# The second attention's scores as one product of 128 partitions a head, and steps of one form side by side

## The reference, cut to what matters

```python
def _attn_ref(q, k, v, p):            # q, k, v: (4, 8, 576, 64); p: (4, 8, 32, 64)
    def sm_attn(qq, kk, vv):
        s = scale * np.matmul(qq, kk.transpose(0, 1, 3, 2))
        s = s - np.max(s, axis=-1, keepdims=True)
        a = np.exp(s)
        a = a / (np.sum(a, axis=-1, keepdims=True) + 1e-09)
        return np.matmul(a, vv)
    p_packed = sm_attn(p, k, v)           # first attention: 32 rows a head
    out = sm_attn(q, p_packed, p_packed)  # second: 576 rows a head against those 32
```

## Time and profile before

| what | value |
|---|---|
| runs, median (lowest to highest of 3) | 1705.7 us (1705.32 to 1707.46) |
| the profiled execution: its time; its span | 1704.49 us; 1702.7 us |
| busy share: PE, PEld, DVE, ACT, POOL | 99%, 88%, 74%, 43%, 74% |
| chain of work that ended last, by engine | PE 94%, POOL 2%, all others 1% or less |
| TensorE's granted clock, 40 slices | 9 in every slice (nine tenths of full or more) |
| waits of PE in the first 110 us | one of 1.1 us for the first data, three of 0.4 to 0.7 for ScalarE's results, one of 0.5 for nothing shown, one of 0.2 |
| DMA issues: k_raw, q_raw, v_raw | 512 KB each, 5.8 to 6.7 us to landing |

### The profile page before, as it was taken

How to read it: one execution, slowest core, us unless ns; L and a number is a source line. 1 busy time by engine, 2 the same in 40 slices (tenths; PEclk the granted TensorE clock), 3 DMA queues, 4 the chain that set the end, 5 groups by cost and what they waited for, 6 DMA issues and landing times.

```text
span 1702.7 us, 28100 instructions
## 1 busy us (share of the span) xinstructions
PE 1691.0 (99%) x10353; PEld 1491.6 (88%) x10353; DVE 1253.8 (74%) x2269; ACT 736.0 (43%) x1666; POOL 1253.5 (74%) x1384
## 2 busy tenths in 40 slices
PE   9999999999999999999999999999999999999999
PEld 7888888888888888888888888888888999889997
DVE  4846645787778787778787878787887677766776
ACT  5644466445444444445444545454532222232222
POOL 1256669987888888778888887888877985399650
PEclk9999999999999999999999999999999999999999
DMA  9431111111111211111112111111100011121101
GB/s 277 124 85 38 41 48 26 38 38 50 38 37 38 61 39 38 39 49 38 38 39 62 38 38 46 42 38 38 50 27 25 26 63 50 38 92 40 62 26 56
DMA packets 78390, 88.32 MB, mean 52 GB/s; under 512 B 8368, under 2 KB 63664, under 8 KB 78256
## 3 DMA queue, kind: packets, MB, share of 16 engines
q1 hardware_dynamic: 78256, 86.54, 18.9%
HBM read 81.81 MB, written 4.72 MB: 51 GB/s over the span
## 4 chain that ended last, share of the span: by engine, by line
PE 94%; POOL 2%; DMA 1%; ACT 1%; DVE 1%; SPq 1%; issue 0%; POOLq 0%; DVEq 0%
PE PS L1651 92%; PE PS L1671 2%; ACT g_raw L892 1%; DMA stage<-moe_w_dram 0%; POOL w_lo L643 0%; PE PS L1881 0%; DMA k_tail<-k_dram 0%; SPq L514 0%; DVE acc L1352 0%; POOL span_late L732 0%; POOL w_hi L641 0%; POOL recombined L716 0%; SPq L538 0%; POOL sums_of_a L724 0%; SPq L531 0%
## 5 line engine op out<-in xcount | busy, mean ns | idle before, releaser
L1651 PE MATMUL PS<-w_hi,h_hi 128*128 128x512 f32 x1440 | 565.7, 393 | 1.2 <-DVE h_lo L1583 0.6
L1651 PE MATMUL PS<-w_lo,h_hi 128*128 128x512 f32 x1440 | 563.4, 391 | 0.0
L1651 PE MATMUL PS<-w_hi,h_lo 128*128 128x512 f32 x1440 | 560.6, 389 | 0.0
L1357 DVE SCALAR_TENSOR_TENSOR acc<-PS,gate,acc 128x512 f32<-128x512 f32 x504 | 378.3, 751 | 178.9 <-PE PS L1651 178.9
L892 ACT ACTIVATE g_raw<-PS 32x256 f32<-32x256 f32 x992 | 373.3, 376 | 12.8 <-PE PS L1651 0.8
L1651 PEld LDWEIGHTS PS<-w_hi,h_lo 128*128 128x128 f32 x1440 | 270.4, 188 | 58.6
L1651 PEld LDWEIGHTS PS<-w_hi,h_hi 128*128 128x128 f32 x1440 | 270.8, 188 | 51.1 <-DVE h_lo L1583 1.1
L1651 PEld LDWEIGHTS PS<-w_lo,h_hi 128*128 128x128 f32 x1440 | 270.9, 188 | 45.8
L1108 ACT ACTIVATE h_hi<-PS 128x576 fp32r<-128x576 f32 x216 | 129.0, 649 | 303.4 <-DVE PS L1493 303.4
L1651 PE MATMUL PS<-a_parts,g_slots 128*128 128x288 f32 x1296 | 225.1, 295 | 0.2 <-POOL g_slots L764 0.2
L1651 PEld LDWEIGHTS PS<-a_parts,g_slots 128*128 128x128 f32 x1296 | 195.7, 188 | 9.6 <-POOL g_slots L764 0.6
(11 more groups left out here) (181 smaller groups left out, 2315.4 us busy)
## 6 DMA issues: line engine op xcount, KB each, us to landing
stage<-moe_w_dram SPq DMA_DIRECT2D x96, 512.0 KB, 4.8
stage<-moe_w_in_dram SPq DMA_DIRECT2D x32, 256.0 KB, 2.8
stage<-moe_w_out_dram SPq DMA_DIRECT2D x16, 512.0 KB, 3.6
k_raw<-k_dram SPq DMA_DIRECT2D x8, 512.0 KB, 6.3
q_raw<-q_dram SPq DMA_DIRECT2D x8, 512.0 KB, 5.8
v_raw<-v_dram SPq DMA_DIRECT2D x8, 512.0 KB, 6.7
out_dram<-acc SPq DMA_DIRECT2D x16, 256.0 KB, 3.7
p_twice<-p_dram SPq DMA_DIRECT2D x8, 64.0 KB, 4.7
```

The lines of the kernel that those rows point to most:

```text
L1357: return nc.vector.scalar_tensor_tensor(out=dst, in0=y, scalar=share, in1=dst, op0=ALU.mult, op1=ALU.add)
L1651: return nc.tensor.matmul(dst, lhsT, rhs, start=start, stop=stop)
```

## The change

- `ppT` grows from 256 to 512 columns, [head, r, 32]. It is zeroed once by GpSimd (`zeros_ready`), and then only rows 0 to 63 of r = 0 and rows 64 to 127 of r = 1 are written, by two copies of ScalarE in place of one. So one product of 128 rows with 64 columns gives both groups of tokens of a head, the zeros keeping them apart: `scores2` issues 8 products a chunk for c = 0, 1 where it issued 16. The tail keeps its form.
- Its results lie in one bank instead of across two, and the bank alternates between 4 and 5, so that a product waits for the scores of two chunks ago.
- `packed`: the second quad of heads begins with its tail product, right behind the first quad's.
- Six steps of TensorE's order are moved.

```diff
-        ppT = [sb(f"ppT{i}", [P, QUADS * P], scope=attn) for i in range(2)]
+        ppT = [sb(f"ppT{i}", [P, H, 2, NPACK], scope=attn) for i in range(2)]
...
-        TR, S1B, S2B, PPB = (0, 1, 6), 2, 4, 7
+        TR, S1B, S2B, PPB = (0, 1, 6), 2, (4, 5), 7
...
+            for i in range(2):
+                nc.gpsimd.memset(ppT[i][:], 0.0).then_inc(zeros_ready, 1)
...
             def packed_values(b):
-                evacuate("pp", b, 0, ppT[b % 2][:], lambda bank_: bank_[:, 0:QUADS * P])
+                unit = UNITS.index(("pp", b, 0))
+                for r in range(2):
+                    rows = slice(r * HALF, (r + 1) * HALF)
+                    done = copy(ppT[b % 2][rows, :, r, :],
+                                full(unit)[rows, 0:QUADS * P].rearrange("d (h n) -> d h n", n=NPACK))
+                done.then_inc(evacuated(unit), 1)
...
+            act.wait_ge(zeros_ready, 2)
             packed_values(0)
...
                 for Q in range(QUADS):
-                    for j in range(RUN + 1):
+                    order = [*range(RUN), RUN] if Q == 0 else [RUN, *range(RUN)]
+                    for j in order:
...
-                elif n:
+                elif b == B - 1:
                     pe.wait_ge(s2_taken, n)
-                copies = 4 if c < NC - 1 else 1
-                for step in range(H):
+                elif n >= 2:
+                    pe.wait_ge(s2_taken, n - 1)
+                for h in range(H):
+                    if c < NC - 1:
+                        last = mm(bank(s2_bank(b, c))[0:tokens, :].rearrange("s (r h n) -> s r h n", r=2, h=H)[:, :, h, :],
+                                  qT[i][:, h, col:col + tokens], ppT[i][:, h, :, :])
+                        continue
                     for r in range(2):
-                        h = step if r else H - 1 - step
                         rows = slice(r * HALF, (r + 1) * HALF)
...
```

The moves in TensorE's order:

```diff
             turn_k(1, 3)
+            turn_k(1, 4)
             packed_gates(0)
-            turn_k(1, 4)
             scores1(1, 0)
...
             turn_k(2, 0)
+            scores2(0, 1)
             turn_q(1, 4)
-            scores2(0, 1)
             turn_k(2, 5)
...
             turn_p(2)
+            turn_k(2, 4)
             turn_k(2, 2)
-            turn_k(2, 4)
             turn_q(2, 5)
             turn_packed(1)
...
             turn_k(3, 5)
+            turn_q(3, 5)
             scores2(2, 0)
-            turn_q(3, 5)
             turn_q(3, 0)
             turn_a(1, 1)
             scores1(3, 1)
+            packed_gates(2)
             turn_q(3, 1)
-            packed_gates(2)
             scores2(2, 1)
```

More of the change, by code:

```diff
@@ L216, in attention_moe_mlp @@
         consts_ready, ones_ready = sem("consts_ready"), sem("ones_ready")
+        zeros_ready = sem("zeros_ready")
         v_in = sem("v_in")
@@ L390, in attention_moe_mlp @@
         TURNED_UNITS = """
[L391 to L394, removed]
+            p00 k00 k02 k01 k05 k03 k04 q02 q03 e00 q00 e01 e02 q01 q04 q05 p10 k12 k11 pp00 k10
+            k13 k14 k15 q15 q12 q13 q10 k20 q14 k25 e10 q11 e11 e12 k23 k21 p20 k24 k22 q25 pp10
+            a00 q23 q24 q22 a01 q21 e20 e21 e22 q20 p30 a02 k32 k31 k30 k34 pp20 k33 a10 k35 q35
+            q30 a11 q31 e30 e31 q32 e32 q33 q34 a12 a20 pp30 a21 a22 a30 a31 a32
         """.split()
@@ L437, in s2_bank @@
         def s2_bank(b, c):
-            return LAST_S2B[c] if b == B - 1 else S2B
+            return LAST_S2B[c] if b == B - 1 else S2B[(b * NC + c) % 2]
         def scores2_of(b, c):
-            at = s2_bank(b, c) * BANK + BANK - H * NPACK
             _, rows, groups = PARTS[c]
+            at = s2_bank(b, c) * BANK + (BANK - H * NPACK if c == NC - 1 else 0)
             return PS[0:rows, at:at + groups * NPACK].rearrange("s (h n) -> s h n", n=NPACK)
@@ L941, in hi_of_packed @@
                 copy(pp_parts[0:HALF, :, b * NPACK:(b + 1) * NPACK],
-                     ppT[b % 2][0:HALF, :].rearrange("d (h n) -> d h n", n=NPACK)).then_inc(pp_hi_ready, 1)
+                     ppT[b % 2][0:HALF, :, 0, :]).then_inc(pp_hi_ready, 1)
             def p_part(b):
@@ L1285, in lo_of_packed @@
                 nc.vector.tensor_tensor(
-                    pp_parts[HALF:P, :, cols], ppT[b % 2][0:HALF, :].rearrange("d (h n) -> d h n", n=NPACK),
+                    pp_parts[HALF:P, :, cols], ppT[b % 2][0:HALF, :, 0, :],
                     pp_parts[0:HALF, :, cols].bitcast(F32), ALU.subtract).then_inc(pp_split, 1)
@@ L1739, in packed @@
                                 weights_, values = e1T[i][0:2 * TAIL, QUADS * RUN + Q, cols], tail[:, h, :]
-                            last = mm(bank(PPB)[out_rows, Q * D:(Q + 1) * D], weights_, values, j == 0, j == RUN)
+                            last = mm(bank(PPB)[out_rows, Q * D:(Q + 1) * D], weights_, values, j == order[0], j == order[-1])
                 last.then_inc(pp_full, 1)
@@ L1755, in scores2 @@
                     pe.wait_ge(s2_taken, n - 1)
-                elif n:
+                elif b == B - 1:
                     pe.wait_ge(s2_taken, n)
-                copies = 4 if c < NC - 1 else 1
-                for step in range(H):
+                elif n >= 2:
[5 more added lines that the diff above has]
+                        continue
                     for r in range(2):
-                        h = step if r else H - 1 - step
                         rows = slice(r * HALF, (r + 1) * HALF)
[L1765 to L1773, removed]
+                        at = (s2_bank(b, c) + 1) * BANK + (h - H) * NPACK
+                        last = mm(PS[r * TAIL:(r + 1) * TAIL, at:at + NPACK], qT[i][rows, h, col:col + tokens],
+                                  ppT[i][rows, h, r, :])
                 last.then_inc(s2_full, 1)
@@ L1833, in packed_gates @@
                         last = mm(bank(GWB)[hq * NPACK:(hq + 1) * NPACK, Q * E:(Q + 1) * E],
-                                  ppT[b % 2][rows, h * NPACK:(h + 1) * NPACK], wg_raw[rows, h // 2, :])
+                                  ppT[b % 2][rows, h, hq % 2, :], wg_raw[rows, h // 2, :])
                 last.then_inc(gw_full, 1)
```

## The result

| | median | runs | range |
|---|---|---|---|
| before | 1705.31 us | 22 | 1703.97 to 1708.38 |
| after | 1710.03 us | 22 | 1705.43 to 1714.96 |

The ratio is 1.0026, with a 95% interval of 1.0020 to 1.0032: slower by just over the 0.2% that can be told apart, and 3 us above the range. The profiled execution of after took 1711.15 us, with a span of 1709.4 against 1702.7.

What follows compares the result with a forecast made beforehand. TensorE, busy 99% of the span, was taken as the bound. Terms of 0.74 + 0.35 + 0.22 + 0.48 − 0.05 − 0.23 + 0.05 + 0.27 = 1.83 us saved gave 1703.9 us, range 1700.0 to 1707.0.

Steps and rivals of the forecast that it cites:

- The sum: All priced changes in the attention's TensorE steps added together: 1.83 us saved.
- a pass of the new form: In the second score product, a full-height pass takes 0.11 us, set by loading 128 weight columns.
- scores2(0, 0) and (1, 1) with their neighbours: Second score products between full-height transpositions: 1.87 us instead of 2.24, saving 0.37 us each, nearly all switches of form.
- wait of q35: Transposition turn_q(3, 5), now ahead of scores2(2, 0), waits 0.57 us for VectorE's copy of k33; net 0.23 us longer.
- k24 and pp10: turn_k(2, 4) before turn_k(2, 2): adjacent tails save 0.27 us of switches, but a wait for ScalarE's copy leaves 0.05.
- each half copy of `ppT`: ScalarE copies in two halves: 0.38 us becomes 0.38 + about 0.26, four times, hidden but for k14.
- if nothing else is late behind it: Condition on the bound: taking TensorE time away can pay in full, provided no other work arrives late.
- No DMA is added or moved: Check of data loads: none changes, and loads that follow TensorE's steps follow them earlier; no cost counted.
- The rival of the clock: Fewer columns moved in scores2 could drop TensorE to 1.2 GHz in the attention; 16 us of it gives 1712; chance 0.05.
- Moved columns as the pace: Rival: moved columns, not weight loads, pace the new product at 0.06 us a pass, giving 1697.5 us; chance 0.10.
- No wait is felt: Rival: q35, pp10 and the early steps cost nothing; 2.8 to 3.2 us saved, about 1702.8 us; chance 0.13.
- The change doesn't do what it says: Rival: switches at each edge, 0.12 us or more a pass, or felt ScalarE copies; about 1706 us; chance 0.12.

Runs made afterwards that it cites:

- the padded version: After with a warm-up of 8 large and 26 small products instead of 10 large, moving later TensorE instructions by 96 records: 1704.46 us, ratio 0.9991.

## Why the prediction was wrong

**The sum was right.** The profile of after moved by 96 records has no pause marked "issue" and no half clock in the attention. It checks the sum, in distances of starts:

| step | forecast | measured |
|---|---|---|
| a pass of the new form | 0.11 | 0.108 |
| scores2(0, 0) and (1, 1) with their neighbours, each less than before | 0.37 | 0.39 |
| scores2(0, 1) with its neighbours | 2.89 | 2.87 |
| scores2(2, 1), gates, scores1 | 3.03 | 2.98 |
| scores2(1, 0) | 2.18 | 2.19 |
| wait of q35 | 0.57 | 0.55 |
| scores2(3, 0) and (3, 1), more than before | 0.05 | 0.09 |
| packed(2), less than before | 0.09 | 0.13 |
| from turn_p(2) to scores1(2, 0) (k24 and pp10), less than before | 0.05 | −0.01 |

Two of the rows behind this, from its timeline, answer to the earlier trace rows: 30.78 − 27.91 = 2.87 us, the tails now side by side.

```profile
27.91 0.60 PE L1684 MATMUL PS<-ident,k_raw 128*128 128x128 f32 x4
28.35 1.90 PE L1661 MATMUL PS<-ppT,acc 128*128 128x64 f32 x16
30.18 0.43 PE L1684 MATMUL PS<-ident,q_tail 32*128 32x32 f32 x4
30.45 0.41 PE L1684 MATMUL PS<-ident,k_tail 32*128 32x32 f32 x4
30.78 0.66 PE L1684 MATMUL PS<-ident,second 128*128 128x128 f32 x4
```

The weight loads of scores2(0, 0) in after show the price of a pass and the missing switches: 27.31 − 25.58 = 1.73 us for 16, with no idle time on either side, where the earlier trace rows have 1.99 and a switch.

```profile
25.20 0.42 PEld L1681 LDWEIGHTS PS<-ident,q_raw 128*128 128x128 f32 x4
25.58 1.87 PEld L1661 LDWEIGHTS PS<-ppT,acc 128*128 128x128 f32 x16
27.31 0.48 PEld L1681 LDWEIGHTS PS<-ident,q_raw 128*128 128x128 f32 x4
```

The Trainium skill, TensorEngine Tiling (Array Packing), "When to Use Tiling", wants two row tiles for a contraction of 64. The prediction worked out from it that here the two forms come out even. The trace agrees but for the switches: 0.108 us a pass here, 0.112 us a pair before.

From the tail k15 to the first product of the experts the padded version takes 50.89 us (23.40 to 74.29), before 53.08 (22.14, to 75.22): 2.19 less. Of these, 0.54 is a pause that before has and this one lacks (66.31 to 67.21, against 65.71 to 66.07), and 1.65 is the change. The sum said 1.83.

One term was mis-sized without harm: each half copy of `ppT` takes 0.378 us (8 of them in after), as long as the whole copy did, so the second adds 0.38 us and not 0.26. It stayed hidden.

**The step that failed** is the sentence "if nothing else is late behind it", which the prediction then checked for banks, copies and data loads only: "No DMA is added or moved". The queue that brings instructions was never looked at, though the page lists it, and before's own timeline has one of its pauses at 66.5 us, which the table ahead of the prediction gives as a wait "for nothing shown". It was taken as a price already paid:

```profile
66.31 0.43 PE L1671 MATMUL PS<-ident,q_tail 32*128 32x32 f32 x4
67.21 0.31 PE L1671 MATMUL PS<-ident,second 64*128 64x64 f32 x2 [0.46 <-issue]
```

It is number 2241 = 193 + 8 × 256. An edit that leaves out 128 passes and their loads moves the later borders, by up to one block; at `packed(1)`, with two chunks of second scores behind it, by 64 records. What stands in place of "nothing else is late" is a stop of 1.73 us in `packed(1)` (2.0 us in the account) and 10.2 us at half clock behind it (4.0 us).

**The rival of the clock** (chance 0.05) named the right mechanism of the loss and the wrong trigger. It put the fall down to fewer columns moved; the runs show it behind a pause. Its price was near: 10.2 us at half clock, halved, are 5.1, and the account shows 4.0 between the starts of scores1(2, 0) and scores1(2, 1), without the first 1.1 us of the stretch. It was to decide from 10.5 us on; the pause's own 2 us made it decide with less. "Against: the clock stays at 1.00 through waits of up to 0.7 us" was true and no evidence for a pause of 1.7 us.

**Moved columns as the pace** (chance 0.10) is refuted by 0.108 us a pass. **No wait is felt** is refuted: q35 waits 0.55 us. **The change doesn't do what it says** is refuted by the table.

**The chances.** 0.08 for slower was too little. What stays open: what sets how long after a border the next packet begins. It was at once before (number 705 at 28.38, the packet at 28.35) and 3.8 to 5.9 us later ahead of the six such pauses of 1.59 us and more. Data loads alone don't explain it. In before the DMA engines were full when that packet began at once, and carried nothing at all while the packet behind number 2241 (66.52) took until 69.32:

```profile
28.00:28.40 0.40, 0.40 (x9) 0.40 (x10) 0.40 (x2) 0.40 (x2) 0.00 (x0) 1.00 1.27 358
66.55:69.30 2.75, 2.29 (x32) 1.59 (x34) 2.30 (x9) 1.43 (x4) 2.00 (x3) 1.00 0.00 0
```

So the place of a harmful border can be found in a trace, but not forecast from the code with what is shown here.

## What to carry to other kernels

Where a stream of short instructions (here 256 in 4.4 us) keeps TensorE full, look in the profile for idle time put down to "issue" in the middle of a loop, and compare it with the packets of the instruction queue; an edit that changes the number of instructions then has to be timed at two or three shifts of the stream (dead instructions at the start), or the shift is measured and not the edit. The versions of after span 7.4 us over shifts alone (those of before 6.1), over four times the change's own worth; before itself had medians of 1704.6 to 1706.3 us in the same sets of runs. The best of after (1704.0 and 1704.5 us) is under before by 0.09%, less than can be told apart.

## What the runs showed of the hardware

- Twelve of the fourteen traces have eighteen pauses of TensorE marked "issue" in the attention, of 0.35 to 2.85 us, all behind the recorded instruction 193 + 256 k (449, 961, 1217, 1473, 1729, 1985, 2241). Each ended 2.3 to 2.7 us after a packet of the instruction queue began: in after 36.07 → 38.60, in before 64.44 → 67.10, in before moved by 160 records 38.76 → 41.17, in after moved by 256 records 35.34 → 37.74.
- In each of the seven traces with an idle time of 1.59 us or more behind 30 us (1.59, 1.73, 1.92, 2.00, 2.27, 2.27, 2.85; the 1.92 for data, the others marked "issue") the granted clock was at half no later than 1.9 us behind its end, and stayed there for 3.4 to 13.7 us although TensorE was busy again. Behind idle times of 0.96 and 1.22 us in the same stretch it stayed at full. In the first 10 us, waits of 0.79 to 1.80 us for `k_raw` came with 3.4 to 6.8 us at half clock in seven traces and with none in two (1.29 and 1.31 us), so these sizes are no sharp bound.
- A full-height product of 128 weight columns paces a pass at 0.108 us with 64 columns moved; with 128 moved no loss could be timed (1704.0 against 1704.5 us).
